# Linear attention on quarters of TensorE's array, with swapped token halves for heads 4 to 7

## Time and profile before

| | |
|---|---|
| median of 3 runs | 402.45 us |
| the profiled execution's own time | 402.08 us |
| its span, first to last instruction | 400.3 us |
| granted TensorE clock, mean | 0.987 |
| TensorE matmul busy | 389.9 us (97%) |
| VectorE, ScalarE, GpSimd busy | 267.6, 219.8, 103.2 us |

### The profile page before, as it was taken

One profiled execution on the slowest core, in us unless ns is written; L12 is line 12 of the kernel. 1 busy time (PEld: TensorE's weight loads), 2 busy tenths in 40 slices (PEclk: granted clock), 3 DMA queues, 4 the chain that ended last, 5 costly groups with the idle time before them and its releaser, 6 DMA issues.

```text
span 400.3 us, 9729 instructions
## 1 busy us (share of the span) xinstructions
PE 389.9 (97%) x3597; PEld 343.8 (86%) x3597; DVE 267.6 (67%) x508; ACT 219.8 (55%) x496; POOL 103.2 (26%) x132
## 2 busy tenths in 40 slices
PE   7799999999999999999999999999999999999997
PEld 6788888888876335479999999999999999999996
DVE  5667777777765731299977766776677677667771
ACT  1587767776776114268745456445645554555441
POOL 5686767676750000046500000000000000000000
PEclk9699999999999899999999999999999999999999
DMA  7899999999999969941002001100200020002002
GB/s 129 177 250 230 230 230 219 228 239 233 227 298 368 423 258 407 405 124 24 0 0 82 2 0 38 40 0 0 79 0 0 0 79 0 0 0 80 0 3 79
DMA packets 87477, 51.87 MB, mean 130 GB/s; under 512 B 76944, under 2 KB 82192, under 8 KB 86416
## 3 DMA queue, kind: packets, MB, share of 16 engines
q1 hardware_dynamic: 87440, 51.38, 44.6%
HBM read 45.86 MB, written 4.72 MB: 126 GB/s over the span
## 4 chain that ended last, share of the span: by engine, by line
PE 88%; DVE 4%; ACT 2%; issue 2%; DMA 2%; SPq 1%; POOL 1%; DVEq 0%; ACTq 0%; POOLq 0%
PE psum L910 16%; PE psum L912 16%; PE psum L911 16%; PE psum L846 6%; PE psum L592 5%; PE psum L624 5%; PE psum L561 4%; PE psum L758 3%; PE psum L632 3%; PE psum L604 3%; PE psum L777 3%; PE psum L615 2%; PE psum L639 2%; ACT scores L1202 1%; DMA u_row<-in_u_dram 1%
## 5 line engine op out<-in xcount | busy, mean ns | idle before, releaser
L912 PE MATMUL psum<-w_out_hi,elu_lo 128*128 128x384 f32 x372 | 125.9, 338 | 0.0
L910 PE MATMUL psum<-w_out_hi,elu_hi 128*128 128x384 f32 x372 | 125.8, 338 | 0.0
L911 PE MATMUL psum<-w_out_lo,elu_hi 128*128 128x384 f32 x372 | 125.3, 337 | 0.0
L1309 ACT ACTIVATE exp_h<-psum 128x512 f32<-128x512 f32 x96 | 57.6, 600 | 100.6 <-PE psum L846 100.6
L1168 DVE SCALAR_TENSOR_TENSOR elu<-psum,neg_part 128x512 f32<-128x512 f32 x96 | 66.3, 690 | 57.0 <-ACT neg_part L1296 57.0
L911 PEld LDWEIGHTS psum<-w_out_lo,elu_hi 128*128 128x128 f32 x372 | 69.8, 188 | 3.8
L910 PEld LDWEIGHTS psum<-w_out_hi,elu_hi 128*128 128x128 f32 x372 | 70.4, 189 | 0.0
L912 PEld LDWEIGHTS psum<-w_out_hi,elu_lo 128*128 128x128 f32 x372 | 69.9, 188 | 0.0
L1160 DVE TENSOR_TENSOR elu_lo<-elu,elu_hi 128x512 fp32r<-128x512 f32 x96 | 67.1, 699 | 0.6
L1296 ACT ACTIVATE neg_part<-exp_h 128x512 f32<-128x512 f32 x96 | 60.1, 627 | 1.7 <-DVE elu L1168 1.4
L1202 ACT ACTIVATE scores<-ident,bonus 128x128 f32<-128x128 f32 x192 | 58.7, 390 | 3.2 <-DVE bonus L953 3.1
(11 more groups left out here) (154 smaller groups left out, 411.7 us busy)
## 6 DMA issues: line engine op xcount, KB each, us to landing
w_sb<-in_moe_w_dram SPq DMA_DIRECT2D x24, 512.0 KB, 4.9
w<-in_moe_w_dram SPq DMA_DIRECT2D x8, 1536.0 KB, 9.1
r_raw<-in_r_dram SPq DMA_DIRECT2D x24, 192.0 KB, 4.7
k_raw<-in_k_dram SPq DMA_DIRECT2D x24, 192.0 KB, 4.8
v_sb<-in_v_dram SPq DMA_DIRECT2D x24, 192.0 KB, 5.5
out_dram<-out_sb SPq DMA_DIRECT2D x24, 192.0 KB, 1.9
w_out_raw<-in_moe_w_out_dram SPq DMA_DIRECT2D x4, 768.0 KB, 11.3
w_in_sb<-in_moe_w_in_dram SPq DMA_DIRECT2D x1, 2304.0 KB, 16.8
```

The source lines that it names most:

```text
L910: pe.matmul(acc, hi, w_out_hi[:, f, :], start=(f == 0), stop=False)
L911: pe.matmul(acc, hi, w_out_lo[:, f, :], start=False, stop=False)
L912: m = pe.matmul(acc, lo, w_out_hi[:, f, :], start=False, stop=(f == KF2 - 1))
L1309: act.activation(exp_h[:, f % 2, :], banks[4 + f % RING][:, :], ACT.Exp).then_inc(exp_done, 1)
```

## The change

- `ident_swap` is an identity whose columns have their halves exchanged. It is a view into a wider constant.
- Each load of r, k or v is three DMAs: heads 0 to 3 as before (128 partitions), and heads 4 to 7 in two DMAs of 64 partitions with the two halves of the tokens exchanged. Semaphore targets go from 16 to 48.
- The transposes of r for heads 4 to 7 use `ident_swap`, so queries stay in order of time while keys and values of these heads are swapped. A second mask serves them, and their decay table is swapped by one copy of ScalarE and one more operation of VectorE.
- The scores are 16 products with 64 stationary columns (8 with 128 moving columns and 8 with 64) in place of 8; the quarter with later keys and earlier queries is left out. The values are 16 products over 64 rows each, in two parts, before and after the scores of the next unit.
- The order on each engine is new: TensorE does state_in, values part 0, scores of the next unit, values part 1, keys times values of the next unit, turn_k, turn_r, turn_x, logits. The other engines follow.
- `slot_early` lies elsewhere in memory. Four warm-up products are larger for two of the banks.

```diff
+            def load(out, x, c, b, loaded):
+                t0, some = c * P, H // 2
+                sp.dma_start(out[:, b, 0:some, 0:D], x[b, t0:t0 + P, 0:some]).then_inc(loaded[b], 16)
+                sp.dma_start(out[0:HP, b, some:H, 0:D], x[b, t0 + HP:t0 + P, some:H]).then_inc(loaded[b], 16)
+                sp.dma_start(out[HP:P, b, some:H, 0:D], x[b, t0:t0 + HP, some:H]).then_inc(loaded[b], 16)
+
             def load_r(c, b):
-                sp.dma_start(r_raw[:, b, :, 0:D], r_dram[b, bass.ds(c * P, P)]).then_inc(r_loaded[b], 16)
+                load(r_raw, r_dram, c, b, r_loaded)
...
             def attend(un, i):
...
-                for a in range(PAIRS):
-                    for two in range(2):
-                        rows = slice(two * HP, two * HP + D)
-                        m = pe.matmul(ps_A[two][:, a, :], k_pair[rows, i, a, :], r_pair[rows, i, a, :],
-                                      start=True, stop=True)
+                for cols, first in ((slice(0, P), 0), (slice(HP, P), 1)):
+                    for n in range(2):
+                        for two in range(2):
+                            for half, a in ((0, n + 2 * first), (1, n + 2 - 2 * first)):
+                                rows, e0 = slice(two * HP, two * HP + D), half * HP
+                                m = pe.matmul(ps_A[two][e0:e0 + HP, a, cols], k_pair[rows, i, a, e0:e0 + HP],
+                                              r_pair[rows, i, a, cols], start=True, stop=True, skip_group_check=True)
...
+            def values(un, b, i, first, part):
+                if part == 0:
+                    pe.wait_ge(scores_ready, 2 * un + 2)
+                else:
+                    pe.wait_ge(y_half_done, un + 1)
+                for q_is_half, cols in ((True, slice(0, P)), (False, slice(HP, P))):
+                    for half in range(2):
+                        two = half if part == 0 else 1 - half
+                        q = half if q_is_half else 1 - half
+                        for e in range(2):
+                            h, rows = 2 * (2 * q + e) + two, slice(half * HP, half * HP + HP)
+                            m = pe.matmul(ps_y[e * HP:e * HP + HP, two, q * P + cols.start:q * P + P],
+                                          v_sb[rows, b, h, :], scores[rows, i, h, cols],
+                                          start=(first and part == 0 and q_is_half),
+                                          stop=(part == 1 and not q_is_half), skip_group_check=True)
+                m.then_inc(y_half_done if part == 0 else y_done, 1)
...
+                    if not first:
+                        state_in(un, b, i, c)
+                    if last:
+                        pe.wait_ge(v_loaded[b], LOADED * CHUNKS)
+                    values(un, b, i, first, 0)
                     if not (last and b == B - 1):
                         attend(un + 1, 1 - i)
+                    else:
+                        turn_x(un - 1, b - 1)
+                    values(un, b, i, first, 1)
+                    if un + 1 < UNITS - B:
...
+                        key_values(un + 1, (b + 1) % B, 1 - i, (un + 1) // B)
+                    if not (last and b >= 2):
+                        turn_k(un + 2)
+                        turn_r(un + 2)
...
+                    if not (last and b >= 2):
+                        turn_x(un, b)
```

More of the change, by code:

```diff
@@ L73, in place @@
             return t
-        ident = place("ident", [P, P], F32)
+        ident_wide = place("ident_wide", [P, P + HP], F32)
+        ident, ident_swap = ident_wide[:, 0:P], ident_wide[:, HP:HP + P]
         ones = place("ones", [P, P], F32)
@@ L111, in attention_moe_ffn_kernel @@
         bonus = place("bonus", [P, 2, H], F32)
-        mask = place("mask", [P, P], F32)
+        mask = place("mask", [P, 2, P], F32)
         wcol = place("wcol", [P, PAIRS], F32)
@@ L571, in turn_k @@
                 wait_for(pe, k_ready, un)
-                turn(banks[1], k_nat[:, un % 2]).then_inc(k_turned, 1)
+                turn(banks[1], k_nat[:, un % 2], ident).then_inc(k_turned, 1)
             def turn_k_first():
@@ L677, in _ @@
             attend(0, 0)
-            pe.wait_ge(r_loaded[1], 16)
-            turn(banks[7], r_raw[:, 1]).then_inc(r_turned, 1)
+            pe.wait_ge(r_loaded[1], LOADED)
+            turn(banks[7], r_raw[:, 1], ident_swap).then_inc(r_turned, 1)
             pe.wait_ge(pads_set, 3)
             turn_k(1)
+            pe.wait_ge(k_scaled, 2)
+            key_values(0, 0, 0, 0)
             def attend_chunk(c, first, last):
@@ L715, in attend_chunk @@
[L715 to L720, removed]
+                    else:
+                        turn_x(un - 1, b - 1)
+                    values(un, b, i, first, 1)
+                    if un + 1 < UNITS - B:
+                        if not first and b == 0:
+                            pe.wait_ge(lT_ready, c)
+                        if not first and b == 1:
+                            pe.wait_ge(logits_ready, c)
+                        key_values(un + 1, (b + 1) % B, 1 - i, (un + 1) // B)
@@ new lines, in attend_chunk @@
+                    if not (last and b >= 2):
+                        turn_k(un + 2)
+                        turn_r(un + 2)
+                    if last and b == 2:
+                        turn_exponentials()
+                    if not (last and b >= 2):
+                        turn_x(un, b)
+                    if not last and b == B - 1:
+                        pe.wait_ge(phi_loaded, 64)
+                        pe.wait_ge(state_summed, min(un + 2, UNITS - B))
+                        chunk_logits_T(c)
@@ L965, in masked @@
                 dve.wait_ge(A_done, un + 1)
[L966 to L968 removed]
+                dve.copy_predicated(scores[:, i, two::2, :].rearrange("p (n a) t -> p n a t", n=2),
+                                    mask[:, :, :].bitcast(U32).unsqueeze(2).broadcast_to([P, 2, 2, P]),
+                                    ps_A[two].rearrange("p (n a) t -> p n a t", n=2)).then_inc(scores_ready, 1)
             def x_to_sbuf(un):
@@ L1020, in attend_chunk @@
                     un, i = c * B + b, b % 2
[L1021 to L1028, removed]
                     if not (last and b == B - 1):
                         masked(un + 1, 1 - i, 0)
[L1031 to L1038, removed]
+                    if not (last and b >= 2):
+                        bonus_of(un + 2, k_raw[:, (un + 2) % B])
                     if not (last and b == B - 1):
                         masked(un + 1, 1 - i, 1)
+                    if un + 1 < UNITS - B:
+                        state_in_sum(un + 1)
                     if not (last and b >= 2):
                         r_to_sbuf(un + 2, banks[0])
-                        bonus_of(un + 2, k_raw[:, (un + 2) % B])
+                    if not (last and b == B - 1):
+                        x_to_sbuf(un)
+                    if not last and b == B - 1:
+                        logits_T_to_sbuf(c)
+                        if c == EARLY_CHUNKS - 1:
+                            early_top()
+                    if not first and b == 0:
+                        logits_to_sbuf(c - 1)
             EARLY, LATE = slice(0, EARLY_CHUNKS * B), slice(EARLY_CHUNKS * B, UNITS)
@@ L1201, in diagonals @@
                 for h in range(two, H, 2):
-                    m = act.activation(scores[:, i, h, :], ident[:, :], ACT.Copy, scale=bonus[:, i, h:h + 1])
+                    m = act.activation(scores[:, i, h, :], ident if h < H // 2 else ident_swap, ACT.Copy,
+                                       scale=bonus[:, i, h:h + 1])
                 m.then_inc(diag_done, 1)
@@ L1217, in _ @@
             k_to_sbuf(1)
+            diagonals(1, 1, 0)
+            diagonals(1, 1, 1)
             def attend_chunk(c, first, last):
@@ L1221, in attend_chunk @@
                     un, i = c * B + b, b % 2
-                    if not (first and b == 0):
-                        y_to_sbuf(un - 1, (b - 1) % B)
+                    if not (last and b == B - 1):
+                        y_to_sbuf(un, b)
+                    if last and b == 1:
+                        early_exponentials()
                     if last and b == 2:
-                        early_exponentials()
-                    if last and b == B - 1:
                         exponentials_to_sbuf()
-                    if not (last and b == B - 1):
-                        diagonals(un + 1, 1 - i, 0)
-                        diagonals(un + 1, 1 - i, 1)
                     if not (last and b >= 2):
                         k_to_sbuf(un + 2)
+                        diagonals(un + 2, i, 0)
+                        diagonals(un + 2, i, 1)
             def early_exponentials():
```

98 lines of the change are left out of this document (55 added, 43 removed).

## The result

The changed kernel takes 457.24 us, median of four runs, against 402.53 for the kernel before on the same chip: a ratio of 1.1345 (95% interval 1.1292 to 1.1398). The forecast was 409.8 us, with 399 to 417 as its range. The direction was right, the size was not: +55 us where +7.8 were forecast, and the time lies far outside the range. The profile shown is of a second run of the same kernel (`again`).

The account below looks back on a forecast made before the run. SP's queue, issuing ten DMAs a unit, was to replace TensorE as the attention's bound: last values end at 134.4 us instead of 126.6, so +7.8 on 402.1 gives 409.8 us; range 399 to 417.

Parts of the forecast that it names:

- The bound: Attention loop: SP's queue, which issues the DMAs, takes 5.18 us a unit, above TensorE's 4.13, and never waits from unit 4.
- The price of an issue: SP's queue: with gap, 0.50 us behind 256 rows and 0.55 behind 512, so one split load takes 1.55 us.
- rival 3: SP's queue: halves of 64 partitions cost 0.625 us each, 6.3 us a unit, about 435 us; 0.09 together with rival 4.
- rival 4: Attention loop: TensorE's clock falls in the new waits, +28 us with half the loop so; 0.09 together with rival 3.
- The hold-ups: SP's queue: issues were priced as not held up; at the last v, 1.2 us of hold-up was counted as gone.
- The sum, term by term: Attention: k of unit 4 issued at 24.9 us, 19 units of 5.18, k of 23 at 123.3, last values end 134.4.
- The end of the attention: Behind the last k: its chain ends at 133.2 us, v lands at 133.4, and values need 1.0 more: 134.4.
- TensorE's part: Attention unit: scores gain 0.36 us, values 0.12, one more break costs 0.17; 0.31 to 0.48 off, to 4.13 us.
- The chain on VectorE: Attention unit: VectorE's work after the scores, the next scores and hand-overs take 4.0 us, under TensorE's 4.13.
- Rival 1: Attention loop: SP's issues are hidden and TensorE sets the pace; 9.2 us comes off, 392.9 us; chance 0.13.

Follow-up runs that it names:

- issue_probe: Kernel before plus 36 unread loads in nine groups of equal DMAs; an issue of 256 rows took 0.47 us with 128 partitions, 0.62 with 64.
- three_full: Changed kernel with three DMAs a load, all of 128 partitions, without the exchange of token halves; 433.48 us, ratio 1.0768.
- one_load: Changed kernel with one DMA for each of r, k and v, without the exchange of token halves; 400.86 us, ratio 0.9986.

## Why the prediction was right and where it failed

*The bound.* Right. SP's queue became the bound with the first unit and never waited for TensorE; the split alone in the old kernel gives 88% of the loss (49.1 of 56.1 us).

*The price of an issue.* This step failed: "behind 256 rows: no row. Between 0.475 and 0.55; I take 0.50". The value rested on the number of rows alone. That is right for 128 partitions (0.47 + 0.04, and 5.25 us a unit against 5.18), but two of three DMAs have 64, and beside them every issue but the first of r costs 0.59 to 0.62. Ten issues are 6.4 us. The right price stood in the text as rival 3 ("halves of 64 partitions are dear to issue", 6.3 us a unit), with 9% between it and rival 4; the bound drawn from the row of 1024 rows was nearly the truth, and the stated range left it out. The prediction also says that the rows agree with the advice against loads on partition halves; no row before shows such a load, and `issue_probe` is the first to price one.

*The hold-ups.* This term is missing: the sum took every issue as one that nothing holds up, and counted a hold-up of before as gone. There was about one of 0.7 us in each unit, which takes the unit from 6.4 to 7.1. In `three_full`, where the price of an issue is as the sum had it, they come to 17.2 us, more than the 7 us between 409.8 and the upper end of the range.

*The sum, term by term.* k of unit 4 was issued at 32.3 us, not 24.9: +7.4. Then 19 units at (166.7 - 32.3) / 19 = 7.07 us for 5.18: +36.0, of which some 23 are the price (6.4 for 5.18) and 13 the hold-ups. From there to the last values' end 16.5 us for 11.1: +5.4. There v of unit 23 landed 13.7 us behind the last k's issue for 10.1, and the work behind it took 2.8 us for 1.0, with the granted clock at 0.50 after TensorE's wait of 4.24 us. Together +48.8, which is 134.4 to 183.2. (7.8 on 402.08 is 409.9, not 409.8.)

*The end of the attention.* The chain from the landing of k to the diagonals went as worked out (168.46 to 174.76). That v would be the later of the two was seen; it came later by more.

*TensorE's part.* Too small in size, and wrong in worth. A unit lost 0.64 us (4.53 to 3.89), where 0.31 to 0.48 were given. The scores gave 0.42 for 0.36; the values only 0.04 for 0.12 (from 65.72 to 66.64 before, now 0.38 and 0.50); and the new order, which was charged with one more break, has one fewer: from state_in to what follows are 0.38 us for 0.60. The chain on VectorE, put at 4.0 us, does not hold a unit of 3.89. Rival 1 gave 392.9 us if the issues were hidden. `one_load` has as few issues as before and takes 400.86. The DMA share of 1.00 stood in the earlier trace rows and was passed over: with one load each, the loads already take what TensorE took.

*Rival 4.* The clock did fall, which the prediction thought it would not: PEclk stands between 7 and 9 in the slices of the loop, with stretches at half clock between those at full, and TensorE is busy 0.70 of the time where 0.79 were assumed. In the loop this cost nothing that shows, for SP, which sets the pace, waited for the engines 0.2 us in all; at the attention's end it is part of the 1.8 us above.

## What to carry to other kernels

Count the issues of each queue as work of an engine: a DMA costs its queue 0.43 to 0.64 us here, whether it moves 48 KB or 512, so cutting a load in three can outweigh any gain on TensorE. Before something is taken off the busiest engine, look at the resource whose share is also at 1.00: here TensorE and the DMAs were level, and 0.6 us a unit off the one was worth nothing. And where no row shows the very shape that the change issues, the far bound belongs inside the range.

## What the runs showed of the hardware that was not expected

- A DMA of 64 partitions costs 0.60 to 0.64 us to issue, where one of 128 with at most 512 rows costs 0.43 to 0.51 (256 rows 0.62 for 0.47, 512 rows 0.64 for 0.51). It also makes its neighbour dearer (w1 behind a half 0.60, behind its own kind 0.43). It is not simply the fewer partitions, for phi's loads, 2 rows in each of 48, cost 0.43; what makes 64 dear no run shows.
- The fetch of a 16 KB page of instructions, one packet of 1.0 to 1.1 us on the average, goes with each of the 67 hold-ups of the table, and each of the 66 fetches with a hold-up that ends shortly after it. More instructions on TensorE gave more of both. How the one holds up the other no run shows.
